# The second layer's gate on 512 columns at a time, with DVE's remainder behind the next reciprocal

## The chip, the core and the metric

The kernel runs on one core of one Trainium2 chip. Five engines run their own instruction streams and meet at semaphores: TensorE (PE in the profile), VectorE (DVE), ScalarE (ACT), GpSimd (POOL), and SyncE (SP), which only issues DMAs. The metric is the device time of one execution in microseconds (us), as the median of three runs.

## What is computed

Sliding-window attention with a few global keys (2 batches, 8 heads, 768 positions, 64 channels) gives x of 1536 x 512. Two feed-forward layers follow, each 512 -> 2048 -> 512. The second one, on which the change acts:

```python
h = x @ w_in                               # 1536 x 2048
h2 = h * h
h3 = h2 * h
P = a[0] + a[1] * h + a[2] * h2 + a[3] * h3
Q = 1.0 + np.abs(b[0]) * np.abs(h) + np.abs(b[1]) * h2
g = P / (Q + 1e-06)                        # the gate
return (g @ w_out).astype(np.float32)
```

All is float32. A matmul operand is split in a high part and a remainder (`_hi`, `_lo`), so each product takes three matmuls: hi·hi, hi·lo, lo·hi.

## The kernel before

The 1536 tokens are 3 blocks of 512 (`TOK`). In each block, each layer goes through 16 steps (`MC`), one for every 128 of the 2048 hidden channels. Layer 2 therefore has 48 steps, numbered u = 0 to 47 here. One step of layer 2 on TensorE is `hidden` (L518: 12 matmuls of 512 columns into one of four PSUM places, `ps_h` twice, `ps_s`, `ps_o`) and `output` (L546: 12 matmuls that add g·w_out to `ps_y`). The order on TensorE is written out by `block_events` (L281): `hidden` of step m+3 stands before `output` of step m (`AHEAD` is 2 for layer 1, 3 for layer 2).

Between the two stands the gate, shared by three engines. A step is cut into two halves of 256 columns (`HALF`), and each half is one unit:

- ACT, `gate2` (L685): reads h from PSUM and makes `h_sq` = h², `numer` = a3·h + a2, `p_low` = a1·h + a0, `q_abs` = |b0|·|h|, and from `h_sq` then `denom` = |b1|·h² + 1 + 1e-6.
- POOL, `gate2` (L1155): `denom` += `q_abs` (L1161), `numer` *= `h_sq` (L1163), `numer` += `p_low` (L1165).
- DVE, `gate2` (L956): the remainder of the same half of the step before (`split2`, L972, `g_lo` = `numer` − `g_hi`, instruction L977), then the reciprocal of `denom` (L967), then the ratio, `numer` *= `denom` (L970).
- ACT, `split2` (L711): `g_hi` = `numer` rounded (L716), issued behind the `gate2` of the same half of the next step.

`numer` and `denom` have four places of 256 columns: two steps. A unit's places are those of the unit four before it, so ACT waits ahead of the unit for `g2_ready`, which DVE raises at L977 (L697: unit u−4 finished). `output` waits for `g2_ready` at each half (L550). The two-half units, the loops (`Fori`) over the first two blocks and the written-out third block all follow `block_events`. Where layer 1 hands over to layer 2, DVE also converts the last weights (L936, L1037) and splits layer 1's result (`end1`, L980).

Of the kernel before, what the change touches and what calls it, by code (L numbers as in the profile page):

```python
# [29 lines left out]
P = 128  # L30
# [3 lines left out]
TOK = 512  # L34
# [27 lines left out]
def build_program(nc, q, k, v, reach, w_in1, w_out1, alpha, w_in2, w_out2, ab, out):  # L62
    ctx = ExitStack()
    with ctx:
# [72 lines left out]
        with ExitStack() as second:  # L137
            stage2 = sb("stage2", [P, 2, KC * PW], F32, second)
            h_sq = sb("h_sq", [P, 2, HALF], F32, second)
            p_low = sb("p_low", [P, 2, HALF], F32, second)  # L140
            q_abs = sb("q_abs", [P, 2, HALF], F32, second)
            numer = sb("numer", [P, 4, HALF], F32, second)
            denom = sb("denom", [P, 4, HALF], F32, second)
# [74 lines left out]
        parts_ready = sem("parts_ready")  # L218
# [259 lines left out]
        def _(pe):  # L478
# [39 lines left out]
            def hidden(layer, blk, m, half, order, wait_w):  # L518

                c = MC * (blk + BLOCKS * layer) + m  # L520
                if m == 0 and layer == 0:

                    pe.wait_ge(x_ready, (blk + 1) * STEPS - 2 + 2 * half)
                if half == 0:
                    if m == 0 and layer == 1:
                        pe.wait_ge(y_read, (blk + 2) * KC)
                    if wait_w:
                        pe.wait_ge(w_ready, 2 * PIECES * layer + hidden_piece(order, m))

                    c2 = MC * blk + m  # L530
                    if layer == 1 and not (isinstance(c2, int) and c2 < 4):
                        pe.wait_ge(h_read, c2 * 2 - 6)
# [117 lines left out]
        def _(act):  # L650
# [34 lines left out]
            def gate2(blk, m, half):  # L685


                u = 2 * MC * blk + 2 * m + half
                r = 2 * (m % 2) + half
                if isinstance(u, int) and u == 0:  # L690
                    act.wait_ge(x_ready, STEPS * BLOCKS)
                    act.wait_ge(g_ready, MC * BLOCKS)
                if not (isinstance(u, int) and u < 2):
                    act.wait_ge(numer_ready, u - 1)
                    act.wait_ge(denom_ready, u - 1)
                if not (isinstance(u, int) and u < 4):
                    act.wait_ge(g2_ready, u - 3)  # L697
                if half == 0:
                    act.wait_ge(h_done, MC * blk + (m + MC * BLOCKS + 1))
                ph = ps_h_at(1, m)[:, half * HALF:(half + 1) * HALF]  # L700
                act.activation(h_sq[:, half, :], ph, ACT.Square).then_inc(parts_ready, 1)
                act.activation(numer[:, r, :], ph, ACT.Identity, scale=ab_sb[:, 3:4],
                               bias=ab_sb[:, 2:3]).then_inc(parts_ready, 1)
                act.activation(p_low[:, half, :], ph, ACT.Identity, scale=ab_sb[:, 1:2],
                               bias=ab_sb[:, 0:1]).then_inc(parts_ready, 1)
                act.activation(q_abs[:, half, :], ph, ACT.Abs, scale=ab_sb[:, 6:7]).then_inc(h_read, 1)
                act.wait_ge(parts_ready, u * 3 + 1)
                act.activation(denom[:, r, :], h_sq[:, half, :], ACT.Identity, scale=ab_sb[:, 7:8],  # L708
                               bias=ab_sb[:, 8:9]).then_inc(denom_square, 1)

            def split2(blk, m, half):  # L711
                u = 2 * MC * blk + (2 * m + half)
                act.wait_ge(ratio_ready, u + 1)
                if half == 0:
                    act.wait_ge(y_done, MC * blk + (m + MC * BLOCKS - 1))
                act.activation(g_hi[:, m % 2, half * HALF:(half + 1) * HALF], numer[:, 2 * (m % 2) + half, :],  # L716
                               ACT.Copy).then_inc(g2_hi_ready, 1)
# [36 lines left out]
            for what, arg in block_events(0, False, "layer"):  # L754
                if what == "g" and arg >= MC:
                    for half in range(2):
                        gate2(0, arg - MC, half)
                        if arg > MC:
                            split2(0, arg - MC - 1, half)
# [4 lines left out]
            with act.Fori(0, BLOCKS - 1) as blk:  # L764
                for what, arg in block_events(1, False, "block"):
                    if what == "g":
                        if arg == MC + AHEAD[1] - 1:
                            end2(blk)
                        for half in range(2):
                            gate2(blk + arg // MC, arg % MC, half)  # L770
                            split2(*before(blk, arg), half)
            for what, arg in block_events(1, False, None):
                if what == "g":
                    for half in range(2):
                        gate2(BLOCKS - 1, arg, half)
                        split2(BLOCKS - 1, arg - 1, half)
                    if arg == MC - 1:
                        for half in range(2):
                            split2(BLOCKS - 1, arg, half)
# [34 lines left out]
        def _(dve):  # L814
# [141 lines left out]
            def gate2(blk, m, half, low_part=True):  # L956

                u, r = 2 * MC * blk + (2 * m + half), 2 * (m % 2) + half
                if isinstance(u, int):
                    if u > 1 and low_part:  # L960
                        split2(*divmod(MC * blk + m - 1, MC), half)
                elif m:
                    split2(blk, m - 1, half)
                else:
                    split2(blk - 1, MC - 1, half)
                dve.wait_ge(denom_ready, u + 1)
                dve.reciprocal(denom[:, r, :], denom[:, r, :]).then_inc(inverse_ready, 1)  # L967
                dve.wait_ge(inverse_ready, u + 1)
                dve.wait_ge(numer_ready, u + 1)
                dve.tensor_tensor(numer[:, r, :], numer[:, r, :], denom[:, r, :], ALU.mult).then_inc(ratio_ready, 1)  # L970

            def split2(blk, m, half):  # L972
                u = 2 * MC * blk + (2 * m + half)
                cut = slice(half * HALF, (half + 1) * HALF)
                dve.wait_ge(ratio_ready, u + 1)
                dve.wait_ge(g2_hi_ready, u + 1)
                dve.tensor_tensor(g_lo[:, m % 2, cut], numer[:, 2 * (m % 2) + half, :],  # L977
                                  g_hi[:, m % 2, cut].bitcast(F32), ALU.subtract).then_inc(g2_ready, 1)
# [33 lines left out]
            for what, arg in block_events(0, False, "layer"):  # L1012
                if what == "g" and arg < MC:
                    gate1(BLOCKS - 1, arg)
                elif what == "g" and arg == MC + 1:

                    gate2(0, 1, 0)
                    split2(0, 0, 1)
                elif what == "g":
                    for half in range(2):  # L1020
                        gate2(0, arg - MC, half)
# [5 lines left out]
                elif what == "end":  # L1027
                    end1(BLOCKS - 1)
                    gate2(0, 1, 1, low_part=False)
# [8 lines left out]
            with dve.Fori(0, BLOCKS - 1) as blk:  # L1038
                for what, arg in block_events(1, False, "block"):
                    if what == "g":  # L1040
                        for half in range(2):
                            gate2(blk + arg // MC, arg % MC, half)
            for what, arg in block_events(1, False, None):
                if what == "g":
                    for half in range(2):
                        gate2(BLOCKS - 1, arg, half)
            for half in range(2):
                split2(BLOCKS - 1, MC - 1, half)
# [98 lines left out]
        def _(pool):  # L1147
# [7 lines left out]
            def gate2(blk, m):  # L1155

                for half in range(2):
                    u, r = 2 * MC * blk + (2 * m + half), 2 * (m % 2) + half
                    top, under = numer[:, r, :], denom[:, r, :]
                    pool.wait_ge(denom_square, u + 1)  # L1160
                    pool.tensor_tensor(under, under, q_abs[:, half, :], ALU.add).then_inc(denom_ready, 1)  # L1161
                    pool.wait_ge(parts_ready, u * 3 + 3)
                    pool.tensor_tensor(top, top, h_sq[:, half, :], ALU.mult).then_inc(numer_high, 1)  # L1163
                    pool.wait_ge(numer_high, u + 1)
                    pool.tensor_tensor(top, top, p_low[:, half, :], ALU.add).then_inc(numer_ready, 1)  # L1165
# [93 lines left out]
```

## Time and profile before

| | us |
|---|---|
| Time, median of 3 runs (lowest, highest) | 700.32 (699.71, 700.37) |
| Span of the profiled execution | 698.6 |
| PE busy | 650.0 |
| DVE busy | 548.3 |
| ACT busy | 379.9 |
| POOL busy | 302.5 |
| First reciprocal of layer 2 (L967) starts at | 410.14 |
| Last one starts at | 687.51 |

The span runs from the first to the last instruction of one execution. The run's time is 1.7 us more than it. In the page, busy time counts an instruction from its start to its end, also while it is held by something inside. A step of layer 2 can be followed by its reciprocals, of which there are two in a step.

### The profile page before, as it was taken

Reading aid. Unit: us, or ns where it says so; the run is one execution under the profiler, and the core shown is the slowest. Engines: PE = TensorE matmul, PEld = TensorE weight load, DVE = VectorE, ACT = ScalarE, POOL = GpSimd, SP = SyncE. Lnnn points to the kernel's source line nnn. Section 1 sums busy time; section 2 is a strip of 40 time slices with the busy share of each in tenths; the row PEclk is TensorE's granted clock in tenths of the full one; section 3 lists DMA queues with packets and bytes.
Section 4 is the critical chain, followed back from the end, with each engine's and each line's share of the span. In section 5 each row is a group of like instructions: output and inputs, shape, how many; then the busy total and the mean of one; then the engine's idle time right before and its main releaser. Section 6 shows DMA issues by size and latency. Waiting matters only on the chain.

```text
span 698.6 us, 10353 instructions
## 1 busy us (share of the span) xinstructions
PE 650.0 (93%) x3072; PEld 508.8 (73%) x3072; DVE 548.3 (78%) x922; ACT 379.9 (54%) x948; POOL 302.5 (43%) x333
## 2 busy tenths in 40 slices
PE   4755899999999999999999998999999999999994
PEld 3533677777787777778888886777777777778873
DVE  8999476676557666654545469999999999999996
ACT  3666143333323333332111167888898888899993
POOL 3455500000000000000444478777777777788882
PEclk8898699999999999999999999999999999999999
DMA  6564111111101101101123210000010000100001
GB/s 203 162 183 144 40 36 44 28 31 49 28 1 30 49 26 30 32 0 61 61 93 114 95 61 0 1 0 1 1 60 0 0 0 0 45 17 1 0 1 64
DMA packets 38937, 31.32 MB, mean 45 GB/s; under 512 B 9008, under 2 KB 33264, under 8 KB 38896
## 3 DMA queue, kind: packets, MB, share of 16 engines
q1 hardware_dynamic: 38896, 30.83, 14.3%
q8 instruction: 19, 0.31, 0.2%
q14 instruction: 22, 0.18, 0.1%
HBM read 27.67 MB, written 3.15 MB: 44 GB/s over the span
## 4 chain that ended last, share of the span: by engine, by line
PE 48%; POOL 25%; DVE 14%; issue 7%; ACT 3%; POOLq 1%; DMA 0%; SPq 0%; DVEq 0%; ACTq 0%
PE ps_h L541 20%; PE ps_y L564 19%; POOL numer L1163 8%; POOL denom L1161 8%; POOL numer L1165 8%; PE ps_s L487 4%; DVE denom L967 3%; PE ps_o L513 3%; PE ps_o L502 2%; DVE xy_raw L913 2%; DVE prob L913 2%; DVE rowmax L893 2%; DVE g_lo L977 1%; DVE den L904 1%; DVE prob L887 1%
## 5 line engine op out<-in xcount | busy, mean ns | idle before, releaser
L967 DVE RECIPROCAL denom<-denom 128x256 f32<-128x256 f32 x96 | 167.3, 1742 | 3.8 <-POOL denom L1161 3.8
L1152 POOL TENSOR_TENSOR win_lo<-stage,win_hi 128x1024 fp32r<-128x1024 f32 x8 | 19.2, 2404 | 276.6 <-DVE win_hi L936 276.6
L541 PE MATMUL ps_h<-xy_hi,win_hi 128*128 (+1 forms) x288 | 119.9, 416 | 0.7 <-DVE xy_lo L925 0.7
L541 PE MATMUL ps_h<-xy_lo,win_hi 128*128 (+1 forms) x288 | 113.8, 395 | 0.0
L541 PE MATMUL ps_h<-xy_hi,win_lo 128*128 (+1 forms) x288 | 113.6, 394 | 0.0
L683 ACT ACTIVATE g_hi<-g 128x512 fp32r<-128x512 f32 x48 | 30.3, 631 | 136.8 <-PE ps_y L564 129.2
L1161 POOL TENSOR_TENSOR denom<-denom,q_abs 128x256 f32<-128x256 f32 x96 | 77.6, 809 | 45.6 <-ACT denom L708 41.6
L566 PE MATMUL ps_y<-wout_hi,g_hi 128*128 128x512 f32 x192 | 79.2, 413 | 10.2 <-DVE g_lo L977 8.3
L953 DVE TENSOR_TENSOR g_lo<-g,g_hi 128x512 fp32r<-128x512 f32 x48 | 33.2, 692 | 66.0 <-ACT g_hi L683 66.0
L564 PE MATMUL ps_y<-g_hi,wout_hi 128*128 128x512 f32 x192 | 80.8, 421 | 0.0
L1163 POOL TENSOR_TENSOR numer<-numer,h_sq 128x256 f32<-128x256 f32 x96 | 77.8, 811 | 0.0
L564 PE MATMUL ps_y<-g_lo,wout_hi 128*128 128x512 f32 x192 | 75.2, 392 | 0.0
L566 PE MATMUL ps_y<-wout_hi,g_lo 128*128 128x512 f32 x192 | 75.1, 391 | 0.0
L564 PE MATMUL ps_y<-g_hi,wout_lo 128*128 128x512 f32 x192 | 75.0, 391 | 0.0
L566 PE MATMUL ps_y<-wout_lo,g_hi 128*128 128x512 f32 x192 | 75.0, 391 | 0.0
L1165 POOL TENSOR_TENSOR numer<-numer,p_low 128x256 f32<-128x256 f32 x96 | 71.2, 742 | 7.5
L665 ACT ACTIVATE probT<-ps_o 128x512 f32<-128x512 f32 x40 | 23.8, 594 | 83.1 <-PE ps_o L502 83.1
L541 PEld LDWEIGHTS ps_h<-xy_hi,win_hi 128*128 128x128 f32 x288 | 54.9, 191 | 14.4 <-issue 2.7
L541 PEld LDWEIGHTS ps_h<-xy_hi,win_lo 128*128 128x128 f32 x288 | 54.8, 190 | 12.0
L541 PEld LDWEIGHTS ps_h<-xy_lo,win_hi 128*128 128x128 f32 x288 | 54.9, 191 | 10.4
L970 DVE TENSOR_TENSOR numer<-numer,denom 128x256 f32<-128x256 f32 x96 | 59.6, 620 | 3.3
L566 PEld LDWEIGHTS ps_y<-wout_hi,g_hi 128*128 128x128 f32 x192 | 36.0, 187 | 33.2 <-DVE g_lo L977 26.1
(128 smaller groups left out, 1331.1 us busy)
## 6 DMA issues: line engine op xcount, KB each, us to landing
stage<-in_w_in SPq DMA_DIRECT2D x8, 512.0 KB, 3.3
stage<-in_w_out SPq DMA_DIRECT2D x8, 512.0 KB, 3.4
qT<-in_q SPq DMA_DIRECT2D x48, 64.0 KB, 2.4
kT<-in_k SPq DMA_DIRECT2D x24, 128.0 KB, 2.3
vv<-in_v SPq DMA_DIRECT2D x24, 128.0 KB, 2.1
out<-xy_raw SPq DMA_DIRECT2D x12, 256.0 KB, 2.2
xy_raw<-in_w_in SPq DMA_DIRECT2D x4, 512.0 KB, 3.8
xy_raw<-in_w_out SPq DMA_DIRECT2D x4, 512.0 KB, 3.6
```

What stands on the lines that cost most here:

```text
L487: mm = pe.matmul(ps_s_at(ab, i)[:, 2 * P * h:2 * P * (h + 1)], qT[:, pair, h, :], kT[:, pair].rearrange("d s t -> d (s t)"), start=True, s ...
L541: mm = pe.matmul(ps_h_at(layer, m), w[:, kc, cut], x[:, blk, kc, :], start=(kc == 0 and n == 0), stop=(kc == KC - 1 and n == 2))
L564: mm = pe.matmul(ps_y[:, j, :], w[:, m, cut], g[:, m % 2, :], **flags)
L566: mm = pe.matmul(ps_y[:, j, :], g[:, m % 2, cut], w[:, m, :], **flags)
L683: act.activation(g_hi[:, m % 2, :], g1[:, :], ACT.Copy).then_inc(g_hi_ready, 1)
L913: dve.tensor_scalar(prob_at(ab, i)[:, h, :], prob_at(ab, i)[:, h, :], rden[:, i % 2, h:h + 1], None, ALU.mult).then_inc(prob_ready, 1)
L953: dve.tensor_tensor(g_lo[:, m % 2, :], g1[:, :], g_hi[:, m % 2, :].bitcast(F32), ALU.subtract).then_inc(g_ready, 1)
L967: dve.reciprocal(denom[:, r, :], denom[:, r, :]).then_inc(inverse_ready, 1)
L970: dve.tensor_tensor(numer[:, r, :], numer[:, r, :], denom[:, r, :], ALU.mult).then_inc(ratio_ready, 1)
L1161: pool.tensor_tensor(under, under, q_abs[:, half, :], ALU.add).then_inc(denom_ready, 1)
L1163: pool.tensor_tensor(top, top, h_sq[:, half, :], ALU.mult).then_inc(numer_high, 1)
L1165: pool.tensor_tensor(top, top, p_low[:, half, :], ALU.add).then_inc(numer_ready, 1)
```

## The change

The gate of layer 2 works on all 512 columns of a step. Every engine has half as many instructions of twice the width. `h_sq`, `p_low` and `q_abs` have one place of 512 columns (two of 256 before), `numer` and `denom` two of 512 (four of 256 before): the bytes are the same. ACT's order in a step becomes square, absolute value, denominator, numerator line, low line. One semaphore for all parts becomes three, and each ACT instruction waits only for what frees its own place. On DVE the order in a step was remainder of the step before, reciprocal, ratio, and is now reciprocal, remainder of the step before, ratio. `output` waits once in a step instead of twice.

```diff
@@ places
-            h_sq = sb("h_sq", [P, 2, HALF], F32, second)
+            h_sq = sb("h_sq", [P, TOK], F32, second)
...
-            numer = sb("numer", [P, 4, HALF], F32, second)
-            denom = sb("denom", [P, 4, HALF], F32, second)
+            numer = sb("numer", [P, 2, TOK], F32, second)
+            denom = sb("denom", [P, 2, TOK], F32, second)
@@ PE, output
-                if layer == 1:
-                    pe.wait_ge(g2_ready, 2 * MC * blk + (2 * m + half + 1))
+                if half == 0 and layer == 1:
+                    pe.wait_ge(g2_ready, MC * blk + (m + 1))
@@ ACT, gate2 (the new one whole)
-                if not (isinstance(u, int) and u < 4):
-                    act.wait_ge(g2_ready, u - 3)
...
+                ph = ps_h_at(1, m)
+                if not (isinstance(u, int) and u == 0):
+                    act.wait_ge(numer_high, u)
+                act.wait_ge(h_done, MC * blk + (m + MC * BLOCKS + 1))
+                act.activation(h_sq[:, :], ph, ACT.Square).then_inc(square_ready, 1)
+                if not (isinstance(u, int) and u == 0):
+                    act.wait_ge(denom_ready, u)
+                act.activation(q_abs[:, :], ph, ACT.Abs, scale=ab_sb[:, 6:7]).then_inc(abs_ready, 1)
                 if not (isinstance(u, int) and u < 2):
...
+                    act.wait_ge(g2_ready, u - 1)
+                act.wait_ge(square_ready, u + 1)
+                act.activation(denom[:, r, :], h_sq[:, :], ACT.Identity, scale=ab_sb[:, 7:8],
+                               bias=ab_sb[:, 8:9]).then_inc(denom_square, 1)
                 act.activation(numer[:, r, :], ph, ACT.Identity, scale=ab_sb[:, 3:4],
...
+                               bias=ab_sb[:, 2:3]).then_inc(line_ready, 1)
+                if not (isinstance(u, int) and u == 0):
+                    act.wait_ge(numer_ready, u)
+                act.activation(p_low[:, :], ph, ACT.Identity, scale=ab_sb[:, 1:2],
+                               bias=ab_sb[:, 0:1]).then_inc(h_read, 1)
@@ DVE
+            def inverse2(blk, m):
+                r = m % 2
+                dve.wait_ge(denom_ready, MC * blk + (m + 1))
                 dve.reciprocal(denom[:, r, :], denom[:, r, :]).then_inc(inverse_ready, 1)
...
+            def split2(blk, m):
...
+                dve.tensor_tensor(g_lo[:, r, :], numer[:, r, :], g_hi[:, r, :].bitcast(F32),
+                                  ALU.subtract).then_inc(g2_ready, 1)
+
+            def gate2(blk, m):
+
+                inverse2(blk, m)
+                split2(blk + (m - 1) // MC, (m - 1) % MC)
+                ratio2(blk, m)
@@ POOL
+                pool.wait_ge(abs_ready, u + 1)
+                pool.wait_ge(denom_square, u + 1)
+                pool.tensor_tensor(under, under, q_abs[:, :], ALU.add).then_inc(denom_ready, 1)
+                pool.wait_ge(line_ready, u + 1)
+                pool.tensor_tensor(top, top, h_sq[:, :], ALU.mult).then_inc(numer_high, 1)
+                pool.wait_ge(numer_high, u + 1)
+                pool.wait_ge(h_read, u + 1)
+                pool.tensor_tensor(top, top, p_low[:, :], ALU.add).then_inc(numer_ready, 1)
```

DVE in the loop over the first two blocks, before, one step and the reciprocal behind it (`g_lo` is the remainder, RECIPROCAL the inverse, `numer<-numer,denom` the ratio):

```order
L977 TENSOR_TENSOR g_lo<-numer,g_hi 128x256 [waits g2_hi_ready,ratio_ready]
L966 REGISTER_ALU
L967 RECIPROCAL denom<-denom 128x256 [waits denom_ready]
L970 TENSOR_TENSOR numer<-numer,denom 128x256 [waits numer_ready,inverse_ready]
L977 TENSOR_TENSOR g_lo<-numer,g_hi 128x256 [waits g2_hi_ready,ratio_ready]
L966 REGISTER_ALU
L967 RECIPROCAL denom<-denom 128x256 [waits denom_ready]
L970 TENSOR_TENSOR numer<-numer,denom 128x256 [waits numer_ready,inverse_ready]
```

DVE at the same place after the change, two steps:

```order
L954 REGISTER_ALU
L955 RECIPROCAL denom<-denom 128x512 [waits denom_ready]
L967 TENSOR_TENSOR g_lo<-numer,g_hi 128x512 [waits g2_hi_ready,ratio_ready]
L961 TENSOR_TENSOR numer<-numer,denom 128x512 [waits numer_ready,inverse_ready]
L954 REGISTER_ALU
L955 RECIPROCAL denom<-denom 128x512 [waits denom_ready]
L967 TENSOR_TENSOR g_lo<-numer,g_hi 128x512 [waits g2_hi_ready,ratio_ready]
L961 TENSOR_TENSOR numer<-numer,denom 128x512 [waits numer_ready,inverse_ready]
```

The remainder of the step before has moved from in front of a reciprocal to behind it.

ACT in the same loop, before, one half and the start of the next (`g2_ready` is raised by DVE's remainder):

```order
L699 REGISTER_ALU [waits g2_ready,denom_ready,numer_ready]
L701 ACTIVATE h_sq<-ps_h 128x256 [waits h_done]
L702 ACTIVATE numer<-ps_h,ab_sb 128x256
L704 ACTIVATE p_low<-ps_h,ab_sb 128x256
L706 ACTIVATE q_abs<-ps_h,ab_sb 128x256
L707 ISA
L708 ACTIVATE denom<-h_sq,ab_sb 128x256 [waits parts_ready]
L716 ACTIVATE g_hi<-numer 128x256 [waits y_done,ratio_ready]
L701 ACTIVATE h_sq<-ps_h 128x256 [waits g2_ready,denom_ready,numer_ready]
```

ACT at the same place after the change, one step:

```order
L697 REGISTER_ALU [waits numer_high]
L698 ACTIVATE h_sq<-ps_h 128x512 [waits h_done]
L701 ACTIVATE q_abs<-ps_h,ab_sb 128x512 [waits denom_ready]
L704 REGISTER_ALU [waits g2_ready]
L705 ACTIVATE denom<-h_sq,ab_sb 128x512 [waits square_ready]
L707 ACTIVATE numer<-ps_h,ab_sb 128x512
L711 ACTIVATE p_low<-ps_h,ab_sb 128x512 [waits numer_ready]
L716 REGISTER_ALU [waits ratio_ready]
L717 ACTIVATE g_hi<-numer 128x512 [waits y_done]
```

The wait for `g2_ready` has moved from in front of the whole gate to in front of the denominator.

## Rows read from the trace of the kernel before

**Rows 1.** Busy time in stretches: loop, third block, its tail, the end

```profile
core 0: us, PE busy (x) PEld busy (x) DVE busy (x) ACT busy (x) POOL busy (x), PEclk, DMA share, GB/s
680.00:691.00 11.00, 7.02 (x28) 4.51 (x27) 10.33 (x13) 5.59 (x14) 6.18 (x9) 1.00 0.00 1
...
690.00:699.00 9.00, 3.02 (x12) 2.18 (x12) 1.85 (x4) 1.36 (x3) 0.00 (x0) 0.80 0.34 123
616.00:676.00 60.00, 59.52 (x262) 48.82 (x261) 59.25 (x66) 56.47 (x133) 52.78 (x67) 1.00 0.00 1
440.00:616.00 176.00, 173.52 (x727) 133.71 (x725) 173.91 (x183) 152.78 (x372) 135.96 (x181) 1.00 0.03 12
```

**Rows 2.** Timeline of one loop step: start, duration (us), engine, instruction, [idle before]

```profile
450.63 1.74 DVE L967 RECIPROCAL denom<-denom 128x256 f32<-128x256 f32 x1
...
452.40 0.42 DVE L970 TENSOR_TENSOR numer<-numer,denom 128x256 f32<-128x256 f32 x1
...
453.08 1.75 DVE L967 RECIPROCAL denom<-denom 128x256 f32<-128x256 f32 x1
453.12 0.73 POOL L1161 TENSOR_TENSOR denom<-denom,q_abs 128x256 f32<-128x256 f32 x1 [1.01 <-ACT denom L708]
...
453.81 0.74 POOL L1163 TENSOR_TENSOR numer<-numer,h_sq 128x256 f32<-128x256 f32 x1
...
454.63 0.74 POOL L1165 TENSOR_TENSOR numer<-numer,p_low 128x256 f32<-128x256 f32 x1
...
454.86 0.78 DVE L970 TENSOR_TENSOR numer<-numer,denom 128x256 f32<-128x256 f32 x1
...
455.57 0.96 DVE L977 TENSOR_TENSOR g_lo<-numer,g_hi 128x256 fp32r<-128x256 f32 x1
...
456.45 1.74 DVE L967 RECIPROCAL denom<-denom 128x256 f32<-128x256 f32 x1
456.72 0.39 ACT L701 ACTIVATE h_sq<-ps_h 128x256 f32<-128x256 f32 x1 [0.62 <-DVE g_lo L977]
```

**Rows 3.** Reciprocal of 256 columns (page: count, busy us, mean ns, idle before)

```profile
L967 DVE RECIPROCAL denom<-denom 128x256 f32<-128x256 f32 x96 | 167.3, 1742 | 3.8 <-POOL denom L1161 3.8
```

**Rows 4.** Reciprocal of 2 columns, view of its line (min/median/max ns)

```profile
L908 DVE RECIPROCAL rden<-den x48: 148/166/167, 11.9 to 308.8; 128x2 f32<-128x2 f32 x48
```

**Rows 5.** DVE's difference on 512 columns, in layer 1 (page)

```profile
L953 DVE TENSOR_TENSOR g_lo<-g,g_hi 128x512 fp32r<-128x512 f32 x48 | 33.2, 692 | 66.0 <-ACT g_hi L683 66.0
```

**Rows 6.** ACT, groups by shape: denominator, `g_hi`, copies from PSUM

```profile
L708 ACT ACTIVATE denom<-h_sq,ab_sb 128x256 f32<-128x256 f32 x96 | 59.3, 618 | 0.0
L716 ACT ACTIVATE g_hi<-numer 128x256 fp32r<-128x256 f32 x96 | 40.6, 423 | 15.9 <-DVE numer L970 14.5
...
L683 ACT ACTIVATE g_hi<-g 128x512 fp32r<-128x512 f32 x48 | 30.3, 631 | 136.8 <-PE ps_y L564 129.2 <-DVE g L946 7.6
...
L727 ACT ACTIVATE xy_raw<-ps_y 128x512 f32 x8 | 4.1, 595 | 0.0
```

**Rows 7.** POOL: 1024 columns (durations min/median/max, ns)

```profile
L1152 POOL TENSOR_TENSOR win_lo<-stage,win_hi x8: 2402/2402/2417, 335.8 to 406.5; 128x1024 fp32r<-128x1024 f32 x8
```

**Rows 8.** Timeline: the first unit's hand-overs ACT to POOL to DVE

```profile
408.68 0.61 ACT L708 ACTIVATE denom<-h_sq,ab_sb 128x256 f32<-128x256 f32 x1
...
409.37 0.74 POOL L1161 TENSOR_TENSOR denom<-denom,q_abs 128x256 f32<-128x256 f32 x1 [0.51 <-ACT denom L708]
...
410.14 1.75 DVE L967 RECIPROCAL denom<-denom 128x256 f32<-128x256 f32 x1 [3.77 <-POOL denom L1161]
```

**Rows 9.** Timeline: first reciprocal of step 3

```profile
433.16 1.74 DVE L967 RECIPROCAL denom<-denom 128x256 f32<-128x256 f32 x1
```

**Rows 10.** Timeline: first reciprocals of steps 35 and 46

```profile
619.42 1.74 DVE L967 RECIPROCAL denom<-denom 128x256 f32<-128x256 f32 x1
...
679.39 1.74 DVE L967 RECIPROCAL denom<-denom 128x256 f32<-128x256 f32 x1
```

**Rows 11.** Timeline: the last matmul of the kernel

```profile
692.74 0.39 PE L566 MATMUL ps_y<-wout_lo,g_hi 128*128 128x512 f32 x1
```

More of the change, by code:

```diff
@@ L138, in build_program @@
             stage2 = sb("stage2", [P, 2, KC * PW], F32, second)
-            h_sq = sb("h_sq", [P, 2, HALF], F32, second)
-            p_low = sb("p_low", [P, 2, HALF], F32, second)
-            q_abs = sb("q_abs", [P, 2, HALF], F32, second)
-            numer = sb("numer", [P, 4, HALF], F32, second)
-            denom = sb("denom", [P, 4, HALF], F32, second)
+            h_sq = sb("h_sq", [P, TOK], F32, second)
+            p_low = sb("p_low", [P, TOK], F32, second)
+            q_abs = sb("q_abs", [P, TOK], F32, second)
+            numer = sb("numer", [P, 2, TOK], F32, second)
+            denom = sb("denom", [P, 2, TOK], F32, second)
         def prob_at(ab, i):
@@ L702, in gate2 @@
-                act.activation(numer[:, r, :], ph, ACT.Identity, scale=ab_sb[:, 3:4],
[L703 to L717, printed above, removed]
+                ph = ps_h_at(1, m)
+                if not (isinstance(u, int) and u == 0):
+                    act.wait_ge(numer_high, u)
@@ L719, in end1 @@
+            def split2(blk, m):
+                act.wait_ge(ratio_ready, MC * blk + (m + 1))
+                act.wait_ge(y_done, MC * blk + (m + MC * BLOCKS - 1))
+                act.activation(g_hi[:, m % 2, :], numer[:, m % 2, :], ACT.Copy).then_inc(g2_hi_ready, 1)
             def end1(blk):
@@ L755, in _ @@
                 if what == "g" and arg >= MC:
[L756 to L759, printed above, removed]
+                    gate2(0, arg - MC)
+                    if arg > MC:
+                        split2(0, arg - MC - 1)
                 elif what == "split" and arg < MC:
@@ L768, in _ @@
                             end2(blk)
-                        for half in range(2):
-                            gate2(blk + arg // MC, arg % MC, half)
-                            split2(*before(blk, arg), half)
+                        gate2(blk + arg // MC, arg % MC)
+                        split2(*before(blk, arg))
             for what, arg in block_events(1, False, None):
                 if what == "g":
-                    for half in range(2):
-                        gate2(BLOCKS - 1, arg, half)
-                        split2(BLOCKS - 1, arg - 1, half)
+                    gate2(BLOCKS - 1, arg)
+                    split2(BLOCKS - 1, arg - 1)
                     if arg == MC - 1:
-                        for half in range(2):
-                            split2(BLOCKS - 1, arg, half)
+                        split2(BLOCKS - 1, arg)
             for j in range(0, KC, 2):
@@ L954, in split1, with ratio2, split2, gate2 @@
                                   ALU.subtract).then_inc(g_ready, 1)
[L956 to L966, printed above, removed]
+            def inverse2(blk, m):
+                r = m % 2
+                dve.wait_ge(denom_ready, MC * blk + (m + 1))
                 dve.reciprocal(denom[:, r, :], denom[:, r, :]).then_inc(inverse_ready, 1)
-                dve.wait_ge(inverse_ready, u + 1)
-                dve.wait_ge(numer_ready, u + 1)
+            def ratio2(blk, m):
+                r = m % 2
+                dve.wait_ge(inverse_ready, MC * blk + (m + 1))
+                dve.wait_ge(numer_ready, MC * blk + (m + 1))
                 dve.tensor_tensor(numer[:, r, :], numer[:, r, :], denom[:, r, :], ALU.mult).then_inc(ratio_ready, 1)
[L972 to L978, printed above, removed]
+            def split2(blk, m):
+                r = m % 2
+                dve.wait_ge(ratio_ready, MC * blk + (m + 1))
+                dve.wait_ge(g2_hi_ready, MC * blk + (m + 1))
+                dve.tensor_tensor(g_lo[:, r, :], numer[:, r, :], g_hi[:, r, :].bitcast(F32),
+                                  ALU.subtract).then_inc(g2_ready, 1)
+            def gate2(blk, m):
+                inverse2(blk, m)
+                split2(blk + (m - 1) // MC, (m - 1) % MC)
+                ratio2(blk, m)
             def end1(blk):
@@ L1014, in _ @@
                     gate1(BLOCKS - 1, arg)
+                elif what == "g" and arg == MC:
+                    inverse2(0, 0)
+                    ratio2(0, 0)
                 elif what == "g" and arg == MC + 1:
-                    gate2(0, 1, 0)
-                    split2(0, 0, 1)
+                    split2(0, 0)
                 elif what == "g":
-                    for half in range(2):
-                        gate2(0, arg - MC, half)
+                    gate2(0, arg - MC)
                 elif what == "split":
@@ L1028, in _ @@
                     end1(BLOCKS - 1)
-                    gate2(0, 1, 1, low_part=False)
+                    inverse2(0, 1)
+                    ratio2(0, 1)
                 elif what == "done":
@@ L1040, in _ @@
                     if what == "g":
-                        for half in range(2):
-                            gate2(blk + arg // MC, arg % MC, half)
+                        gate2(blk + arg // MC, arg % MC)
             for what, arg in block_events(1, False, None):
                 if what == "g":
[L1045 to L1048, printed above, removed]
+                    gate2(BLOCKS - 1, arg)
+            split2(BLOCKS - 1, MC - 1)
             for j in range(1, KC, 2):
@@ L1155, in gate2 @@
             def gate2(blk, m):
[L1157 to L1165, printed above, removed]
+                u, r = MC * blk + m, m % 2
+                top, under = numer[:, r, :], denom[:, r, :]
+                pool.wait_ge(abs_ready, u + 1)
[6 more added lines that the diff above has]
+                pool.tensor_tensor(top, top, p_low[:, :], ALU.add).then_inc(numer_ready, 1)
             done = [0]
```

16 lines of the change are left out of this document (5 added, 11 removed).

## Prediction

> **What bounds the kernel now.** I read the stretches first [rows 1]. The change touches layer 2 alone, from about 410 us on. In the loop (440 to 616 us) DVE is busy 173.9 of 176 us, but PE is busy too, so the stretches don't decide it; the distance of the reciprocals does. A loop step takes 456.45 − 450.63 = 5.82 us [rows 2]: one step is reciprocal, ratio, remainder, twice. From step 3 (433.16, [rows 9]) to step 35 (619.42, [rows 10]) it is 186.26 / 32 = 5.82 as well. PE could go faster: in the third block, where it is busy 59.5 of 60 us with 24 matmuls a step [rows 1], steps 35 to 46 run at (679.39 − 619.42) / 11 = 5.45 us [rows 10]. So PE's floor is 5.45, or 2.72 for 12 matmuls. DVE sets the loop, PE the third block.
>
> What fills DVE's 5.82? Two reciprocals of 1.74 that nothing stretches, and four operations on two tensors that take 0.42 us at best, and 0.78 and 0.96 where a POOL instruction runs beside them (454.86 and 455.57 against 452.40, [rows 2]). So some 0.9 us a step is DVE being held. The trace shows it as busy.
>
> **Widths.** A 512-column instruction isn't in the gate yet, so each is made from two widths. Reciprocal: 1742 ns at 256 [rows 3], 166 at 2 [rows 4], so 6.2 ns a column and 3.34 us at 512. Ratio and remainder: 0.69 [rows 5]. ACT: 631 − 423 = 208 ns for 256 more columns [rows 6]; denominator 618 + 208 = 0.83. POOL: 0.74 at 256 [rows 2], 2.40 at 1024 [rows 7], so 0.55 per 256 more and 1.29 at 512. Upper end of each is twice its 256-column time: 3.48, 0.84, 1.24, 1.48.
>
> Counted as work, this is a gain: DVE has 3.34 + 0.69 + 0.69 = 4.7 us a step, less than PE's 5.45. POOL has 3 × 1.29 = 3.9. Nobody but PE would be full.
>
> **The change, as a cycle.** Two edits meet. Step u's `denom` and `numer` lie in the places of step u−2, so ACT's denominator of u waits for the remainder of u−2 (`g2_ready` ≥ u−1). And that remainder now stands behind the reciprocal of u−1 on DVE. Follow one turn, with 0 where the remainder of u−2 ends:
> - ACT sees it after 0.19: the remainder at 455.57 ends at 456.53, ACT's waiting square starts at 456.72 [rows 2]. Lower end 0.04, as nothing less is seen.
> - ACT makes the denominator of u: 0.83, to 1.02. Its square and absolute value are done by then (below).
> - POOL starts 0.08 later (409.29 to 409.37, [rows 8]) and adds `q_abs`: 1.29, to 2.39.
> - DVE starts the reciprocal of u 0.03 later (410.11 to 410.14, [rows 8]): 3.34, to 5.76. What DVE had left, the ratio of u−1, ran from 0 to 0.62; DVE then idles 1.8 us.
> - The remainder of u−1 follows without a wait on the reciprocal. Instructions back to back overlap by 0.08 (the remainder at 455.57 ends at 456.53, the next reciprocal starts at 456.45), dependent ones are 0.03 apart (450.63 + 1.74 to 452.40). I take −0.05, then 0.69: to 6.40.
>
> That is the turn, and each step needs one: **6.40 us a step** against 5.82 and 5.45. Before, the same place was four units old, the wait was for a remainder that stood in front of two reciprocals still to come, and ACT and POOL had these two, 3.5 us, to hide in. Now there is none between the remainder of u−2 and the reciprocal of u, because the one of u−1 is already over.
>
> What lies beside the turn, and its slack. POOL's two numerator operations follow its first: starts 0.69 and 0.82 apart at 256 [rows 2], 1.25 and 1.38 at 512, so they end at 1.10 + 2.63 + 1.29 = 5.02, 0.7 before DVE's remainder starts. DVE is no longer held: the 0.9 us vanishes, but only into idle time. ACT: line, low line and `g_hi` end near 2.9, square of u+1 starts when POOL's product ends (about 3.7), absolute value ends near 5.0: 1.5 before its next denominator. At a block's end, twice, ACT has four PSUM copies of 2.1 us in all to do [rows 6] once that block's last `output` is through (2.72 into the turn): copies to about 5.0, square and absolute value to 6.2, just in time for 6.6. PE needs 5.45 of 6.40 and waits 0.95 at each `output`. PE's second wait in a step, which is gone, costs and gives nothing while PE waits anyway. No DMA moves.
>
> The row shows an operation of DVE stretched from 0.42 to 0.96 beside POOL. The Trainium skill ("SBUF — State Buffer", section "SBUF: two separate sides") says that DVE instructions with two SBUF inputs and GpSimd's share a port pair as an exclusive lock, so that the later one waits for the whole of the other. By that rule a POOL instruction of 512 columns in DVE's way would cost up to 1.29 instead of 0.7, and the turn would be up to 7.7 if it met one; by the slack above it meets none.
>
> **The sum.** Hand-over: the first reciprocal starts at 410.14 [rows 8] and the one of step 3 at 433.16 [rows 9]. For steps 0 to 2 DVE is then held 3 × 0.9 us less and has 3 × (3.48 − 3.34) = 0.4 less of reciprocal, against about 1 us of a new wait (the remainder of step 0 for ACT's `g_hi`, behind a 512-column gate of step 1). I put the reciprocal of step 3 at 431.0 (429.5 without that wait, 433.2 as now). Then 44 turns to step 47: 44 × 6.40 = 281.6, to 712.6. Its reciprocal, remainder of 46, ratio, ACT's `g_hi`, remainder of 47: 3.34 + 0.64 + 0.61 + 0.67 + 0.74, to 718.6. `output` of 46 starts when its remainder is done, 716.6, and ends at 719.3; `output` of 47 follows, its last matmul starts 11 × 0.227 = 2.5 later, 721.8. From there to the end of the span it is 698.6 − 692.74 = 5.9 now [rows 11], and stays. Span 727.7, against 698.6. The run's median lies 1.7 above its span: **729.4 us**, 4.2% slower.
>
> **Rivals.**
> - *Faster: the gate runs at its work, not at the cycle.* The Trainium skill ("VectorE: DVE Perf Modes", section "The TRN2 errata — SBUF-src ops pay a fixed extra latency per instruction") advises tiles of 512 elements or more, so that the fixed part is paid once. For this to win here, the wait for `g2_ready` would have to be satisfied early, and nothing could set the pace but PE's 5.45 [rows 1]: 729.4 − 44 × 0.95 = 687.6. For it: 4.7 us of DVE work. Against: both ends of the wait are in the order of instructions, and the reciprocal alone is half of the turn. It decides once ACT, POOL and the hand-overs between them take under 1.3 us; their rows give 2.4. Chance 4%.
> - *Slower still: widths double and POOL collides.* If reciprocal and POOL's addition take twice their 256-column time, the turn is 6.40 + 0.14 + 0.19 = 6.73: 744. If ACT and the remainder double too, 7.35: 771. If POOL's last operation ends after DVE's reciprocal (0.7 us late), it holds the remainder and adds its overhang. Against: each slope comes from two rows. Chance 8% for above 742.
> - *TensorE's clock.* PE now waits 0.95 us each step. Before, gaps of about that size each 2.7 us left the granted clock at 1.00 (680 to 691 us), and 0.80 shows only once PE has ended [rows 1]. At 1.2 GHz a step would take PE twice 5.45 by estimate, 4.5 more than a turn: were that so in 4 or 5 of the 44 steps, 20 us more, 749. Chance 4%.
>
> **Numbers.** Forecast (6.2 to 6.68 us a turn, 720 to 742): 84%. The lower end is a turn with 0.04 for the first wait and full overlap, 6.22, and 429.5 at the start: 720. What a measurement can tell here is about 0.2%, 1.4 us; within it I leave 2%, as the pace would have to fall by chance on 5.7. Faster 4%, slower 94%. Range 720 to 742, which leaves out the faster rival, the 744 and beyond, and the clock.
>
> **What will show it.** Reciprocals 6.40 us apart in all three blocks, the third no faster. DVE idle about 1.8 us a step in front of each reciprocal, released by POOL's addition; ACT's denominator waiting for DVE's remainder; POOL's addition waiting for ACT's denominator; ratio and remainder at 0.69 each, never held; PE waiting 0.95 for the remainder at each output. It is wrong if ACT's denominator starts without waiting for the remainder, if reciprocals lie 5.5 apart, or if the reciprocal takes other than 3.3 us.

## The result and the profile after

The changed kernel takes 724.2 us (median of four executions; 723.54 to 725.86) against 700.32: a ratio of 1.034, 95% interval 1.033 to 1.036. The profiled execution took 725.86, its span is 724.1, the last reciprocal starts at 707.90 where it was 687.51.

Busy time fell on every engine of the gate and the time rose. This is the first part of the page; the kernel before had DVE 548.3, ACT 379.9 and POOL 302.5:

```profile
PE 655.1 (90%) x3072; PEld 510.6 (71%) x3072; DVE 494.2 (68%) x778; ACT 325.2 (45%) x660; POOL 266.3 (37%) x189
```

The step against [rows 2], from the timeline of the changed kernel (start, duration in us, engine, instruction, [idle before, releaser]):

```profile
501.02 3.35 DVE L955 RECIPROCAL denom<-denom 128x512 f32<-128x512 f32 x1 [1.80 <-POOL denom L1155]
...
502.35 0.60 ACT L698 ACTIVATE h_sq<-ps_o 128x512 f32<-128x512 f32 x1 [0.94 <-POOL numer L1157]
502.85 0.68 ACT L701 ACTIVATE q_abs<-ps_o,ab_sb 128x512 f32<-128x512 f32 x1
504.29 0.63 DVE L967 TENSOR_TENSOR g_lo<-numer,g_hi 128x512 fp32r<-128x512 f32 x1
504.84 0.68 DVE L961 TENSOR_TENSOR numer<-numer,denom 128x512 f32<-128x512 f32 x1
505.03 0.82 ACT L705 ACTIVATE denom<-h_sq,ab_sb 128x512 f32<-128x512 f32 x1 [1.50 <-DVE g_lo L967]
...
505.99 1.30 POOL L1155 TENSOR_TENSOR denom<-denom,q_abs 128x512 f32<-128x512 f32 x1 [2.38 <-ACT denom L705]
...
507.33 3.35 DVE L955 RECIPROCAL denom<-denom 128x512 f32<-128x512 f32 x1 [1.81 <-POOL denom L1155]
```

Read it as a chain: the remainder ends at 504.92, ACT's denominator starts at 505.03, POOL's addition follows it at 505.99, the reciprocal follows that at 507.33, the next remainder follows the reciprocal. Each of the three hand-overs is named in the brackets of the one that waits, and each engine in the ring idles. Reciprocals lie 507.33 − 501.02 = 6.31 us apart. The list of waits, 440 to 700 us (us in total, times, longest), says the same for all steps:

```profile
POOL denom L1155 <- ACT denom L705: 96.7, 41, 2.4
DVE denom L955 <- POOL denom L1155: 75.0, 42, 1.8
ACT denom L705 <- DVE g_lo L967: 60.1, 40, 1.5
PEld ps_y L568 <- DVE g_lo L967: 39.0, 41, 1.0
ACT h_sq L698 <- POOL numer L1157: 36.1, 39, 1.0
```

Three engines wait in a ring, some 40 times each, once a step: that is how a cycle looks in such a list. In the kernel before, DVE's reciprocals waited for nobody in that stretch.

### The profile page after: what moved, and what is told of

The parts are those of the page before. It is cut to its first block, busy times and chain, and to the rows that moved or that the text cites. A ratio compares the mean times of both kernels' runs of the same rounds, so it can differ in the third digit from the quotient of the medians.

```text
span 724.1 us, 9497 instructions
## 1 busy us (share of the span) xinstructions
PE 655.1 (90%) x3072; PEld 510.6 (71%) x3072; DVE 494.2 (68%) x778; ACT 325.2 (45%) x660; POOL 266.3 (37%) x189
## 4 chain that ended last, share of the span: by engine, by line
PE 47%; POOL 24%; DVE 13%; ACT 7%; issue 7%; DMA 0%; POOLq 0%; SPq 0%; DVEq 0%; ACTq 0%
PE ps_h L543 20%; PE ps_y L566 18%; POOL numer L1157 8%; POOL denom L1155 8%; POOL numer L1160 8%; ACT denom L705 5%; PE ps_s L489 4%; DVE g_lo L967 4%; PE ps_o L515 3%; PE ps_o L504 2%; DVE xy_raw L909 2%; DVE prob L909 2%; DVE rowmax L889 1%; DVE den L900 1%; PE ps_y L568 1%
## 5 line engine op out<-in xcount | busy, mean ns | idle before, releaser
L955 DVE RECIPROCAL denom<-denom 128x512 f32<-128x512 f32 x48 | 160.9, 3352 | 82.6 <-POOL denom L1155 82.6
L568 PE MATMUL ps_y<-wout_hi,g_hi 128*128 128x512 f32 x192 | 81.8, 426 | 29.7 <-DVE g_lo L967 29.7
L1155 POOL TENSOR_TENSOR denom<-denom,q_abs 128x512 f32<-128x512 f32 x48 | 62.7, 1306 | 109.3 <-ACT denom L705 109.3
L705 ACT ACTIVATE denom<-h_sq,ab_sb 128x512 f32<-128x512 f32 x48 | 39.2, 817 | 65.5 <-DVE g_lo L967 65.3
L1160 POOL TENSOR_TENSOR numer<-numer,p_low 128x512 f32<-128x512 f32 x48 | 62.6, 1304 | 3.8
L1157 POOL TENSOR_TENSOR numer<-numer,h_sq 128x512 f32<-128x512 f32 x48 | 63.2, 1316 | 0.0
```

The lines of the kernel that those rows point to most:

```text
L568: mm = pe.matmul(ps_y[:, j, :], g[:, m % 2, cut], w[:, m, :], **flags)
L705: act.activation(denom[:, r, :], h_sq[:, :], ACT.Identity, scale=ab_sb[:, 7:8], bias=ab_sb[:, 8:9]).then_inc(denom_square, 1)
L1155: pool.tensor_tensor(under, under, q_abs[:, :], ALU.add).then_inc(denom_ready, 1)
L1157: pool.tensor_tensor(top, top, h_sq[:, :], ALU.mult).then_inc(numer_high, 1)
L1160: pool.tensor_tensor(top, top, p_low[:, :], ALU.add).then_inc(numer_ready, 1)
```

## Experiments

All ratios are against the kernel before (median 700.15 beside the first four kernels, 699.62 beside the last three).

**The wait that closes the ring, alone.** ACT's denominator waits for the ratio of step u−2, the last reader of its place; the line behind it takes the wait for the remainder.

```diff
                 if not (isinstance(u, int) and u < 2):
-                    act.wait_ge(g2_ready, u - 1)
+                    act.wait_ge(ratio_ready, u - 1)
                 act.wait_ge(square_ready, u + 1)
                 act.activation(denom[:, r, :], h_sq[:, :], ACT.Identity, scale=ab_sb[:, 7:8],
                                bias=ab_sb[:, 8:9]).then_inc(denom_square, 1)
+                if not (isinstance(u, int) and u < 2):
+                    act.wait_ge(g2_ready, u - 1)
```

> The changed kernel, with one wait moved on ACT: the denominator of step u waits for the ratio of step u-2 (the last reader of its place), and only the numerator line behind it waits for the remainder of u-2. DVE's order, the widths and all work stay. Theory (the cycle remainder of u-2, ACT denominator, POOL addition, reciprocal of u sets the 6.30 us step): the cycle opens, DVE has about 4.7 us of work a step, so TensorE's 5.45 us sets the step in all three blocks: 431.8 + 44 x 5.45 and the same end, some 37 us less than the changed kernel, 686 to 690 us. Rival (wide instructions and their hand-overs are what costs, whatever the wait): the step stays above 6.2 us, 720 us or more.

Measured: 692.24 us (691.89 to 692.87), ratio 0.989 (0.987 to 0.991). 32 us came back from one wait, at the same widths, instruction counts and DVE order. The ring is the cause. But 692 is above the 686 to 690 expected. The timeline of this kernel:

```profile
504.86 0.62 DVE L969 TENSOR_TENSOR g_lo<-numer,g_hi 128x512 fp32r<-128x512 f32 x1
504.96 1.67 POOL L1157 TENSOR_TENSOR denom<-denom,q_abs 128x512 f32<-128x512 f32 x1 [0.75 <-ACT denom L705]
505.40 1.78 DVE L963 TENSOR_TENSOR numer<-numer,denom 128x512 f32<-128x512 f32 x1
...
506.59 1.74 POOL L1159 TENSOR_TENSOR numer<-numer,h_sq 128x512 f32<-128x512 f32 x1
507.10 3.34 DVE L957 RECIPROCAL denom<-denom 128x512 f32<-128x512 f32 x1
...
510.72 0.63 ACT L698 ACTIVATE h_sq<-ps_s 128x512 f32<-128x512 f32 x1
...
514.09 3.35 DVE L957 RECIPROCAL denom<-denom 128x512 f32<-128x512 f32 x1 [2.51 <-POOL denom L1157]
```

The ratio takes 1.78 instead of 0.68, and POOL's operations 1.67 and 1.74 instead of 1.30: without the idle time they meet, and a step takes 5.50 (501.60 to 507.10 in the same view), with DVE busy 60.00 of the 60 us from 616 on. DVE's fullness alone doesn't show that DVE sets the 5.50, because being held counts as busy, and the list of waits (440 to 680 us) has a second ring in it:

```profile
POOL denom L1157 <- ACT denom L705: 36.2, 43, 3.1
...
ACT h_sq L698 <- POOL numer L1159: 23.9, 40, 1.1
```

POOL's product lets ACT's next square start, then come absolute value, denominator, POOL's addition and again the product: in the third block one product starts at 669.03 and the next at 674.52, 5.49 us later. Two of its links are POOL operations that DVE holds. This run can't tell DVE's load from this ring.

Where a block ends, one step takes 7.0 (507.10 to 514.09): ACT's four copies out of PSUM stand in front of its gate.

**The order alone undone.** DVE in the old order, remainder, reciprocal, ratio, on 512 columns.

```diff
             def gate2(blk, m):
 
-                inverse2(blk, m)
                 split2(blk + (m - 1) // MC, (m - 1) % MC)
+                inverse2(blk, m)
                 ratio2(blk, m)
```

> The changed kernel with DVE's old order: remainder of the step before, then reciprocal, then ratio, all on 512 columns. Theory: the remainder of u-2 is ready before the reciprocal of u-1, so ACT and POOL are hidden behind that; DVE now waits for ACT's rounding between ratio and remainder (0.04 + 0.62 + 0.1 us), 3.35 + 0.7 + 0.75 + 0.63 = 5.4 us a step, up to 6.0 if POOL's operations hold ratio and remainder: 690 to 715 us. Rival (width alone makes it slow): 724 us or more.

Measured: 708.6 us (707.0 to 709.23), ratio 1.012 (1.009 to 1.014). So the change with DVE's old order costs 8 us (this kernel has ACT's new order too), and DVE's new order on top another 16. Its timeline:

```profile
501.62 0.94 DVE L967 TENSOR_TENSOR g_lo<-numer,g_hi 128x512 fp32r<-128x512 f32 x1 [0.77 <-ACT g_hi L717]
...
502.48 3.34 DVE L955 RECIPROCAL denom<-denom 128x512 f32<-128x512 f32 x1
...
505.85 0.86 DVE L961 TENSOR_TENSOR numer<-numer,denom 128x512 f32<-128x512 f32 x1
...
506.74 0.63 ACT L717 ACTIVATE g_hi<-numer 128x512 fp32r<-128x512 f32 x1 [1.93 <-DVE numer L961]
...
507.48 0.93 DVE L967 TENSOR_TENSOR g_lo<-numer,g_hi 128x512 fp32r<-128x512 f32 x1 [0.77 <-ACT g_hi L717]
```

DVE now waits 0.77 for ACT's rounding each step and is held by POOL in ratio and remainder (0.86 and 0.94): 5.86 us (502.48 to the reciprocal at 508.34). That wait is what the new order was able to hide, and did: it is gone in the changed kernel. It hid 0.8 us and closed a ring that costs more.

Not all of the 24 us lie in the steps. From the reciprocal of step 3 to the last one it is 254.4 us in the kernel before, 259.1 here and 276.2 in the changed kernel: the new order adds 17 us to the steps. Behind the last reciprocal the profiled executions take 11.1, 15.8 and 16.2 us. So some 5 us of the change come from the end, with either order. In the changed kernel TensorE's last 24 matmuls wait for the remainder of step 46 and start at 711.85, so the last matmul starts 9.3 us behind the last reciprocal, where it was 5.2 (687.51 to 692.74); the rest lies behind it.

**The order alone done**, in the kernel before, on halves of 256.

```diff
-                if isinstance(u, int):
-                    if u > 1 and low_part:
-                        split2(*divmod(MC * blk + m - 1, MC), half)
-                elif m:
-                    split2(blk, m - 1, half)
-                else:
-                    split2(blk - 1, MC - 1, half)
                 dve.wait_ge(denom_ready, u + 1)
                 dve.reciprocal(denom[:, r, :], denom[:, r, :]).then_inc(inverse_ready, 1)
+                if isinstance(u, int):
+                    if u > 1 and low_part:
+                        split2(*divmod(MC * blk + m - 1, MC), half)
+                elif m:
+                    split2(blk, m - 1, half)
+                else:
+                    split2(blk - 1, MC - 1, half)
```

> The kernel before with the new order alone: halves of 256 columns, DVE takes the remainder behind the reciprocal. Places are those of four units before, so there are two reciprocals between a remainder and the reciprocal that needs it. Theory: no tight cycle; a step of 5.45 to 5.82 us, 688 to 701 us. Rival (the remainder behind the reciprocal costs by itself, since TensorE gets it later): clearly slower than before, 710 us or more.

Measured: 700.35 us, ratio 1.001 (0.999 to 1.002): no difference. With four places of 256 the same order does no harm. Its reciprocals mostly lie 2.81 us apart, 5.63 a step, but eight of the steps behind step 3 take 6.1 to 6.6, for a reason that was not traced. That makes 5.76 a step from 3 to 35 (431.09 to 615.37) and 5.72 from 35 to 46 (to 678.33), where the kernel before has 5.82 and 5.45. Step 3 starts 2.1 us sooner, the loop gives back another 2.0, the third block costs 3.0 and the end the rest.

**One ACT instruction more, on the ring and beside it.** h is copied to an unused place; what is computed stays. On the ring:

```diff
+            unused = sb("unused", [P, TOK], BF16, second)
...
                 if not (isinstance(u, int) and u < 2):
                     act.wait_ge(g2_ready, u - 1)
+                if not (isinstance(u, int) and u == 0):
+                    act.wait_ge(unused_done, u)
+                act.activation(unused[:, :], ph, ACT.Copy).then_inc(unused_done, 1)
                 act.wait_ge(square_ready, u + 1)
```

> The changed kernel with one more ACT instruction a step, a copy of h (128x512) to an unused place, between the wait for the remainder and the denominator: on the cycle. Theory: each turn grows by the copy's 0.49 us, 46 x 0.49 = 22.5, to 747 us, step 6.8 us. Rival (ACT is 45 to 57% busy and not on the path): 724 us.

Measured: 742.38 us (two executions, 742.36 and 742.41), ratio 1.060 (1.058 to 1.063), a step of 6.70 us.

Beside the ring, the same three lines right behind the square:

```diff
                 act.activation(h_sq[:, :], ph, ACT.Square).then_inc(square_ready, 1)
+                if not (isinstance(u, int) and u == 0):
+                    act.wait_ge(unused_done, u)
+                act.activation(unused[:, :], ph, ACT.Copy).then_inc(unused_done, 1)
```

> The changed kernel with the same additional ACT instruction as in the run with the copy on the cycle (h copied to an unused place, 128x512), but right behind the square, ahead of the wait for the remainder. ACT waits 1.5 us there in every step of the changed kernel. Theory: nothing moves, a step of 6.30 us and 724 us, with ACT's wait for the remainder 1.0 instead of 1.5 us. Rival (any additional ACT work or a later absolute value delays POOL): a step of 6.7 us as on the cycle, 742 us.

Measured: 726.37 us (724.69 to 726.41), ratio 1.038 (1.036 to 1.040), a step of 6.30 us. The same work cost 18 us in one place and 2 in the other. Both kernels' rows, first on the ring, then beside it:

```profile
507.50 0.63 DVE L972 TENSOR_TENSOR g_lo<-numer,g_hi 128x512 fp32r<-128x512 f32 x1
...
508.16 0.60 ACT L708 ACTIVATE unused<-ps_o 128x512 bf16<-128x512 f32 x1 [1.43 <-DVE g_lo L972]
508.65 0.81 ACT L710 ACTIVATE denom<-h_sq,ab_sb 128x512 f32<-128x512 f32 x1
```

```profile
503.75 0.69 ACT L706 ACTIVATE q_abs<-ps_o,ab_sb 128x512 f32<-128x512 f32 x1
504.73 0.63 DVE L972 TENSOR_TENSOR g_lo<-numer,g_hi 128x512 fp32r<-128x512 f32 x1
...
505.47 0.82 ACT L710 ACTIVATE denom<-h_sq,ab_sb 128x512 f32<-128x512 f32 x1 [1.02 <-DVE g_lo L972]
```

Beside the ring it only shortens ACT's wait, from 1.50 to 1.02. On the ring it adds 0.40 a step, not its 0.49: the copy starts 0.03 behind the remainder (508.13 to 508.16), where the denominator had started 0.11 behind it, so the later start of the waiting instruction falls away. Beside the ring the slack is used up at the two block ends: the reciprocals lie 6.62 us apart there (520.33 to 526.95) instead of 6.30, 0.6 us in all. The rest of the 2 us is within what executions of one kernel differ by: the changed kernel's span 2.3 us, and the two profiled ones are only 0.5 apart (726.36 and 725.86).

**Toward a version that beats both.** ACT's four copies moved inside the gate of that step, behind its denominator, on top of the moved wait:

```diff
                                bias=ab_sb[:, 8:9]).then_inc(denom_square, 1)
+                if between is not None:
+                    end2(between)
...
-                        if arg == MC + AHEAD[1] - 1:
-                            end2(blk)
-                        gate2(blk + arg // MC, arg % MC)
+                        gate2(blk + arg // MC, arg % MC, between=blk if arg == MC + AHEAD[1] - 1 else None)
```

> The kernel with the denominator waiting for the ratio alone (692.2 us), and ACT's four PSUM copies at a block's end put inside the gate of the third step of the next block, between its denominator and its line, instead of ahead of the gate. In the kernel without this, two steps take 7.0 and 6.9 us instead of 5.50, where DVE waits 2.5 us for POOL behind a late denominator. Theory (ACT's copies delay the denominator): both long steps shrink to 6.0 or less, 2 to 3 us less in all, about 690 us. Rival (those steps are long because TensorE finishes the block then): 692 us.

Measured: 690.82 us (689.54 to 691.23), ratio 0.987 (0.986 to 0.989). The long steps are gone (5.50 and 5.67), and the last reciprocal starts 2.8 us sooner (672.25 against 675.03). The time fell by 1.4 only. The other half went to TensorE's clock at the end. Here are the start of `output` of step 46 and the stretch from there to the last matmul (columns as in [rows 1], granted clock third from the end), first with the moved wait alone, where the start of `output` of step 45 stands ahead, then with the later copies:

```profile
673.49 0.50 PE L568 MATMUL ps_y<-wout_hi,g_hi 128*128 128x512 f32 x1 [2.48 <-DVE g_lo L969]
...
678.97 0.50 PE L568 MATMUL ps_y<-wout_hi,g_hi 128*128 128x512 f32 x1 [0.88 <-DVE g_lo L969]
...
678.97:684.70 5.73, 5.73 (x24) 4.42 (x24) 1.93 (x3) 1.23 (x2) 0.00 (x0) 1.00 0.01 3
```

```profile
676.20 0.50 PE L568 MATMUL ps_y<-wout_hi,g_hi 128*128 128x512 f32 x1 [2.44 <-DVE g_lo L969]
...
676.20:683.60 7.40, 7.35 (x24) 5.57 (x24) 1.93 (x4) 1.24 (x3) 0.00 (x0) 0.77 0.01 2
```

From there to the last matmul's start it is 5.36 us in the one (to 684.33) and 6.96 in the other (to 683.16), for the same 24 matmuls: 1.6 us. With the moved wait alone the clock fell too, but earlier, behind the wait at 673.49 (granted 0.50 to 0.51 from 674 to 677). It slowed `output` of 45 there, and TensorE still waited 0.88 for the next remainder, so it cost nothing.

Then, on top of both, the absolute value ahead of the square:

```diff
-                if not (isinstance(u, int) and u == 0):
-                    act.wait_ge(numer_high, u)
                 act.wait_ge(h_done, MC * blk + (m + MC * BLOCKS + 1))
-                act.activation(h_sq[:, :], ph, ACT.Square).then_inc(square_ready, 1)
                 if not (isinstance(u, int) and u == 0):
                     act.wait_ge(denom_ready, u)
                 act.activation(q_abs[:, :], ph, ACT.Abs, scale=ab_sb[:, 6:7]).then_inc(abs_ready, 1)
+                if not (isinstance(u, int) and u == 0):
+                    act.wait_ge(numer_high, u)
+                act.activation(h_sq[:, :], ph, ACT.Square).then_inc(square_ready, 1)
```

> As the run with the later copies, and ACT takes the absolute value ahead of the square, which waits for POOL's product. The denominator of the next step is then ready about 0.5 us sooner on ACT. If DVE's step of 5.50 is set by the ratio that POOL's addition holds (1.77 instead of 0.67 us), the addition starts sooner and holds the remainder in place of the ratio: a step between 5.45 (TensorE's floor) and 5.6, 687 to 693 us. If the late denominator were what sets 5.50, TensorE's 5.45 in every step, 2 us less than the run with the later copies.

Measured: 686.98 us (686.78 to 687.48), ratio 0.982 (0.981 to 0.984), the fastest here: 13 us below the kernel before, 37 below the changed one. Steps alternate between 5.50 and 5.2 to 5.4, with 6.1 behind the block ends, 5.41 on average from 457.43 to 598.11 (26 steps). TensorE sets the pace now: its `output` of step 3 starts at 441.07 and that of step 44 at 664.11, 41 steps of 5.44 us, the 5.45 that the prediction took for its floor. The reciprocals can lie closer as long as the gate still catches up with TensorE. The stretch of the loop (same columns as [rows 1]):

```profile
440.00:616.00 176.00, 176.00 (x778) 145.75 (x777) 173.62 (x98) 132.23 (x204) 135.98 (x98) 1.00 0.03 12
```

Two DVE operations are still held in turn, here the ratio, then the remainder of the next step:

```profile
504.11 1.77 DVE L963 TENSOR_TENSOR numer<-numer,denom 128x512 f32<-128x512 f32 x1
...
509.06 1.49 DVE L969 TENSOR_TENSOR g_lo<-numer,g_hi 128x512 fp32r<-128x512 f32 x1
```

So the remainder is held in place of the ratio in every other step, as the first of the two expectations has it, and TensorE's pace comes in every step, as the second has it. The edit took the absolute value out of the second ring and moved POOL's addition at once, so what had set the 5.50, DVE being held or that ring, stays open.

## Why the prediction was right, and by how much it missed

The mechanism was the one named: the remainder of u−2, ACT's denominator, POOL's addition, the reciprocal, in a ring without slack. One wait moved opened it, and one instruction lengthened it in one place and not in another. The ring's terms, predicted and measured (504.29 to 510.60):

| us | predicted | measured |
|---|---|---|
| remainder's end to ACT | 0.19 | 0.11 |
| denominator | 0.83 | 0.82 |
| ACT to POOL | 0.08 | 0.14 |
| POOL's addition | 1.29 | 1.30 |
| POOL to DVE | 0.03 | 0.04 |
| reciprocal | 3.34 | 3.35 |
| overlap | −0.05 | −0.08 |
| remainder | 0.69 | 0.63 |
| turn | 6.40 | 6.31 |

The widths, made from two rows each, hold to 0.01 us. What was mis-sized are the seams, and the remainder: its 0.69 came from a row in which it waits for another engine each time [rows 5], while right behind another DVE instruction it is shown with 0.63. Small errors partly cancel: the first hand-over is 0.08 and the remainder 0.06 too long, the overlap 0.03 too small, the hand-over to POOL 0.06 too short. The page's group for the reciprocals confirms the long term:

```profile
L955 DVE RECIPROCAL denom<-denom 128x512 f32<-128x512 f32 x48 | 160.9, 3352 | 82.6 <-POOL denom L1155 82.6
```

The sum step by step: the reciprocal of step 3 starts at 431.75 (431.0 predicted). The 44 turns take 707.90 − 431.75 = 276.2, 6.28 each, not 281.6: 5.4 us less. "The third no faster" was wrong: there a turn is 6.22, as ACT's denominator follows the remainder by 0.03 to 0.04:

```profile
642.74 0.63 DVE L967 TENSOR_TENSOR g_lo<-numer,g_hi 128x512 fp32r<-128x512 f32 x1
...
643.40 0.82 ACT L705 ACTIVATE denom<-h_sq,ab_sb 128x512 f32<-128x512 f32 x1 [1.50 <-DVE g_lo L967]
```

That block is written out with constant step numbers, so it needs no register instruction like the one that the order of ACT shows at this wait in the loop. That this is what saves the 0.08 is not shown. The prediction had a lower end of 0.04 for this term and should have split it by block.

The last matmul starts at 717.20 (721.8), and the span ends 6.9 behind it (5.9), so 724.1 against 727.7. The prediction let the 5.9 stay; in the other wide kernels it is 5.8 to 6.4, and what makes it differ was not traced. The remaining 1.7 is the profiled execution, which was the slowest of four. So here too errors partly cancel: 0.8 us too little up to step 3 and 1.1 behind the last reciprocal, 5.4 too much in the turns and 1.7 in the step from span to median, 5.2 too much in all.

Three figures beside the sum don't come out of their terms. Without the new wait step 3 would start at 430.0, not 429.5 (433.16 − 2.7 − 0.4). With ACT and the remainder doubled too the turn is 7.29, not 7.35 (6.73 + 0.41 + 0.15), or 769 us. And the faster rival would need ACT, POOL and their hand-overs under 1.4 us, not 1.3 (5.45 − 3.34 − 0.03 − 0.64). The upper end of 6.68 us a turn has no working. None of them moves the forecast.

The cover held where it was claimed. The ratio took 0.68 and the remainder 0.63, never held in the loop; POOL's last operation ended 0.7 before the remainder (502.32 + 1.29 = 503.61 against 504.29); the block ends fitted. PE's wait is 0.95 by the sum, and 39.0 / 41 = 0.95 for its weight loads in the list; that the two agree to the digit is luck, since the turn that came leaves 6.31 − 5.45 = 0.86. On the rivals: the faster one is what the ring was hiding. It needed the wait to be satisfied early, and with the wait moved it came out, at 5.50 and not 5.45: POOL and DVE meet again and the second ring leaves no slack, and the rival's price left both out. The trace agrees with the rule cited for it (the Trainium skill, "VectorE: DVE Perf Modes", section "The TRN2 errata — SBUF-src ops pay a fixed extra latency per instruction": a wide tile pays the fixed part once) as far as it goes: a reciprocal of 512 takes 3.35 against 2 × 1.74 [rows 3]. The clock rival did not come: granted 1.00 from 440 to 700 us with PE waiting each step.

POOL and DVE meeting shows in the kernel with the moved wait: the ratio there starts at 505.40, POOL's addition ends at 506.63, the ratio ends at 507.18, so its own work begins about when POOL's ends. The Trainium skill ("SBUF — State Buffer", section "SBUF: two separate sides") calls the shared port pair an exclusive lock. These rows agree but for some 0.15 us at the edges: the ratio lies beside the addition for 1.23 us and is 1.10 longer. They show it both ways: POOL's next operation starts at 506.59, lies beside the ratio for 0.59 and takes 1.74, 0.44 longer. No run here took POOL's operation away, so that the lock is the cause is argued from these times, not shown by an experiment.

## What to carry to other kernels

When units are made wider in the same memory, the number of places halves, and a wait for "the unit four before" becomes one for "two before"; moving the releasing instruction behind a long one at the same time can leave no slack. Before such a change, write down the ring for each reused place (who frees it, who fills it, what lies between on each engine) and add it up: here a few rows gave 6.40 where 6.31 came, while busy times promised a gain. Then let each writer wait for the last reader of its own place and not for the end of the whole unit: that one line was worth 32 us.

## What the runs showed of the hardware that was not expected

At the very end PE waited 3.19 us for one remainder, and its granted clock fell behind that wait (stretches of the changed kernel; columns as in [rows 1], PEclk is third from the end):

```profile
703.00:705.50 2.50, 0.00 (x0) 0.00 (x0) 2.50 (x2) 1.11 (x2) 1.25 (x1) 1.00 0.00 0
705.50:709.00 3.50, 3.35 (x8) 2.68 (x9) 1.79 (x3) 2.67 (x4) 2.42 (x2) 0.51 0.00 0
709.00:718.00 9.00, 6.94 (x29) 5.06 (x28) 5.15 (x6) 1.61 (x3) 1.39 (x2) 1.00 0.04 12
```

For about 3 us matmuls took 0.63 us instead of 0.39 (the lower level, 1.2 GHz). It cost nothing there, as the next remainder came later still: PE waited 1.65 for it at 711.85. In the kernel with the later copies it did cost: the fall came behind the wait of 2.44 at 676.20, and `output` of 46 and 47 took 1.6 us more. The same kernel's wait of 2.50 at 670.70 left the clock at 1.00, while a wait of 2.48 in the kernel with the moved wait alone (673.49) was followed by a fall; what decides between them is not shown. The short waits at each `output` of the changed kernel (0.56 in PE's own rows, 0.95 for its weight loads), every 6.3 us, left the clock at 1.00.
